# The last two row blocks of a two-stage MLP computed together, with seven products of matrix quarters in place of eight

## The reference, cut to what matters

```python
x = attention(rotate(q), rotate(k), v)      # (4, 576, 512): 4 batches, 8 heads of 64
h = x.transpose(0, 2, 1) @ U @ V            # rank 32, mixes the 576 positions
u = x + h.transpose(0, 2, 1)
ch = np.maximum(u @ w_ch1, 0.0) @ w_ch2     # 512 -> 2048 -> 512
return u + ch
```

## Time and profile before

| | us |
|---|---|
| median of 3 runs | 745.0 (744.42 to 745.64) |
| the profiled execution | 744.88 |
| its span in the profile | 743.1 |
| TensorE busy | 713.4 (96%) |
| VectorE, ScalarE, POOL busy | 405.4 (55%), 440.7 (59%), 463.5 (62%) |
| mean granted TensorE clock | 0.991 of full speed |

### The profile page before, as it was taken

How to read it: one execution, slowest core, us unless ns; L and a number is a source line. 1 busy time by engine, 2 the same in 40 slices (tenths; PEclk the granted TensorE clock), 3 DMA queues, 4 the chain that set the end, 5 groups by cost and what they waited for, 6 DMA issues and landing times.

```text
span 743.1 us, 12350 instructions
## 1 busy us (share of the span) xinstructions
PE 713.4 (96%) x4314; PEld 644.1 (87%) x4314; DVE 405.4 (55%) x677; ACT 440.7 (59%) x951; POOL 463.5 (62%) x335
## 2 busy tenths in 40 slices
PE   9899986999999999999999999899999999999997
PEld 4888875999997879999999988899899889999986
DVE  4899997555657775344444566676565441112111
ACT  2988875666767666566565665676666334333331
POOL 3999865384958664674946967639333255656563
PEclk9999997899999999999999999999999999999999
DMA  7976684528493538348274374462523253434342
GB/s 207 242 215 178 185 255 119 161 94 236 110 245 106 161 133 244 132 140 251 86 214 177 104 209 149 147 187 79 159 73 103 100 183 124 168 128 170 127 171 71
DMA packets 73757, 117.84 MB, mean 159 GB/s; under 512 B 27040, under 2 KB 27168, under 8 KB 71904
## 3 DMA queue, kind: packets, MB, share of 16 engines
q1 hardware_dynamic: 73472, 116.68, 52.2%
q10 hardware_dynamic: 224, 0.36, 0.2%
HBM read 80.15 MB, written 9.44 MB: 121 GB/s over the span
## 4 chain that ended last, share of the span: by engine, by line
PE 72%; DVE 8%; ACT 7%; POOL 6%; issue 5%; DMA 1%; POOLq 0%; SPq 0%; ACTq 0%; DVEq 0%
PE ps L1151 25%; PE ps L1167 22%; PE ps L1050 7%; PE ps L1064 7%; PE ps L1085 5%; DVE negmax L877 2%; POOL raw L588 2%; PE ps L1019 2%; ACT prob L720 2%; POOL raw L589 1%; ACT pth L731 1%; ACT w2h L784 1%; PE ps L1133 1%; ACT w1h L780 1%; POOL raw L598 1%
## 5 line engine op out<-in xcount | busy, mean ns | idle before, releaser
L655 POOL TENSOR_TENSOR w2l<-w2u,w2h 128x512 fp32r<-128x512 f32 x96 | 124.0, 1291 | 223.5 <-ACT w2h L784 223.5
L978 DVE SCALAR_TENSOR_TENSOR htl<-ps,hth 128x384 fp32r<-128x384 f32 x96 | 53.5, 558 | 177.5 <-ACT hth L791 177.0
L877 DVE TENSOR_REDUCE negmax<-ps 128x1 f32<-128x576 f32 (+1 forms) x160 | 120.2, 751 | 49.4 <-PE ps L1050 42.4
L731 ACT ACTIVATE pth<-ps 128x512 fp32r<-128x512 f32 (+1 forms) x156 | 87.7, 567 | 81.6 <-PE ps L1085 80.3
L1151 PE MATMUL ps<-ub,w1h 128*128 128x384 f32 x384 | 133.2, 347 | 1.1 <-DVE htl L978 0.6
L720 ACT ACTIVATE prob<-ps,negmax 128x576 f32<-128x576 f32 (+1 forms) x160 | 118.0, 738 | 27.3 <-DVE negmax L877 27.1
L1151 PE MATMUL ps<-ub,w1l 128*128 128x384 f32 x384 | 129.7, 338 | 0.0
L1151 PE MATMUL ps<-utl,w1h 128*128 128x384 f32 x384 | 129.5, 337 | 0.0
L649 POOL TENSOR_TENSOR w1l<-w1u,w1h 128x512 fp32r<-128x512 f32 x96 | 124.1, 1293 | 5.8 <-ACT w1h L780 5.8
L791 ACT ACTIVATE hth<-ps 128x384 fp32r<-128x384 f32 x96 | 47.0, 490 | 130.6 <-PE ps L1151 130.3
L1050 PE MATMUL ps<-stack 128*128 128x288 f32 x620 | 112.9, 304 | 7.6 <-ACT prob L720 7.2
(11 more groups left out here) (84 smaller groups left out, 1137.5 us busy)
## 6 DMA issues: line engine op xcount, KB each, us to landing
w1u<-in_w SPq DMA_DIRECT2D x96, 256.0 KB, 2.6
w2u<-in_w SPq DMA_DIRECT2D x96, 256.0 KB, 2.6
stack<-raw SPq DMA_DIRECT2D x60, 288.0 KB, 4.4
raw<-in_qk SPq DMA_DIRECT2D x14, 1152.0 KB, 5.3
stack<-raw SPq DMA_DIRECT2D x60, 144.0 KB, 4.0
v2u<-in_v SPq DMA_DIRECT2D x16, 320.0 KB, 4.2
ubu<-scratch_u SPq DMA_DIRECT2D x18, 256.0 KB, 3.6
out<-ubu SPq DMA_DIRECT2D x18, 256.0 KB, 2.4
```

What stands on the lines that cost most here:

```text
L655: nc.gpsimd.tensor_tensor(w2l[:, at], w2u[:, at], w2h[:, at], ALU.subtract).then_inc(w2_lo, 1)
L731: nc.scalar.activation(pt_of(g)[0][rows, keys, queries], source, ACT.Copy).then_inc(pt_hi, 1)
L877: nc.vector.tensor_reduce(negmax[0:WT[t], t:t + 1], scores_of(n, WT[t]), AX.XY, ALU.max, negate=True).then_inc(maxed, 1)
```

## The change

Blocks 4 and 5 are taken together, and their 16 inner blocks in HP = 8 pairs. Pair 0 is computed as before, four ups (`plain`) and the downs. In pairs 1 to 7 the 256 x 512 weights A and the 512 x 768 rows B of u are cut into 2 x 2 quarters (128 x 256 and 256 x 384), and the four up products are made from seven products of quarters and sums of quarters in place of eight, by these formulas:

- S1 = A21 + A22, S2 = S1 - A11, S3 = A11 - A21, S4 = A12 - S2 (weights, by POOL, `s_sums`, for each pair);
- T1 = B12 - B11, T2 = B22 - T1, T3 = B22 - B12, T4 = B21 - T2 (rows of u, by DVE, `sum_t`, once; they serve all seven pairs);
- P1 = A11 B11, P2 = S2 T2, P3 = A12 B21, P4 = S3 T3, P5 = S1 T1, P6 = A22 T4, P7 = S4 B22 (this is the order in which they are made);
- U2 = P1 + P2, C11 = P1 + P3, U3 = U2 + P4, C22 = U3 + P5, U4 = U2 + P5, C21 = U3 + P6, C12 = U4 + P7 (by DVE, `wide_add`).

Every product is 2 x 3 = 6 matmuls of 384 columns (`product`), and alternates between banks 5 and 7. Behind P1 to P7 stand 2, 2, 2, 2, 2, 1 and 1 downs of the pair before (`DOWNS_BEHIND`); the twelve downs of the last pair come at the end. The downs add up in six banks. ACT rounds the quarters (`round_a`, 128x768), the sums (`round_s`, 128x1024), and the T (`round_t`, 128x768 each); POOL makes the `lo` parts of quarters and sums (`a_rest`, `s_rest`), DVE those of the T (`rest_t`, 128x768 each). The relu and its `lo` part (`wide_relu`, `wide_rest`) now read C from SBUF for pairs 1 to 7; for pair 0 they read the bank. Sums, T and C lie in buffers of the attention that are free by then. Weights are loaded once for both blocks. The first pair's sums and quarters are made in slots 166 and 168. STEPS is now 64, so `MLP_REST` has three parts, the downs of step 63.

```diff
+LONE = NB - 2
+STEPS = LONE * FB
+HP = FB // 2
+PRODUCTS = ("a11", "s2", "a12", "s3", "s1", "a22", "s4")
+DOWNS_BEHIND = (2, 2, 2, 2, 2, 1, 1)
+FIRST_PAIR = NTILES + 6
...
+            def s_sums(k):
+                a21, a22, a11, a12 = (place("w_raw", k % 2, QUARTER * i, QUARTER) for i in range(4))
+                s1, s2, s3, s4 = (place("s_raw", None, QUARTER * i, QUARTER) for i in range(4))
+                pool.wait_ge(pair_loaded[k % 2], 32 * ((k + 1) // 2))
...
+                nc.gpsimd.tensor_tensor(s1, a21, a22, ALU.add).then_inc(s_sum, 1)
+                nc.gpsimd.tensor_tensor(s3, a11, a21, ALU.subtract).then_inc(s_sum, 1)
+                pool.wait_ge(s_sum, 4 * (k - 1) + 1)
+                nc.gpsimd.tensor_tensor(s2, s1, a11, ALU.subtract).then_inc(s_sum, 1)
+                pool.wait_ge(s_sum, 4 * (k - 1) + 3)
+                nc.gpsimd.tensor_tensor(s4, a12, s2, ALU.subtract).then_inc(s_sum, 1)
...
             for x in MLP_REST:
                 mlp(*x)
+            w2_rest(STEPS)
+            w2_rest(STEPS + 1)
+            for k in range(1, HP):
+                w2_rest(STEPS + 2 * k)
+                if k + 1 < HP:
+                    s_sums(k + 1)
+                    a_rest(k + 1)
+                    s_rest(k + 1)
+                w2_rest(STEPS + 2 * k + 1)
...
+            wide_relu(0, 0, 0)
+            round_w2(STEPS)
+            round_t(T3)
+            round_t(T2)
+            wide_relu(0, 0, 1)
+            wide_relu(0, 1, 0)
+            round_w2(STEPS + 1)
+            wide_relu(0, 1, 1)
+            for k in range(1, HP):
+                if k == 1:
+                    round_t(T1)
+                wide_relu(k, 0, 0)
+                if k == 1:
+                    round_t(T4)
+                round_w2(STEPS + 2 * k)
+                if k + 1 < HP:
+                    round_a(k + 1)
+                wide_relu(k, 1, 1)
+                if k + 1 < HP:
+                    round_s(k + 1)
+                wide_relu(k, 1, 0)
+                wide_relu(k, 0, 1)
+                round_w2(STEPS + 2 * k + 1)
...
+            sum_t(T3)
+            wide_rest(0, 0, 0, 1)
+            sum_t(T2)
             for x in MLP_REST:
                 mlp(*x)
+            wide_rest(0, 0, 1, 2)
+            rest_t(T3, 1)
+            rest_t(T2, 2)
+            wide_rest(0, 1, 0, 3)
+            sum_t(T1)
+            wide_rest(0, 1, 1, 4)
+            for k in range(1, HP):
+                wide_add(k, 1, "p1", None)
+                if k == 1:
+                    rest_t(T1, 3)
+                wide_add(k, 2, "u2", "p1")
+                if k == 1:
+                    sum_t(T4)
+                wide_add(k, 3, "c11", "p1")
+                if k == 1:
+                    rest_t(T4, 4)
+                wide_add(k, 4, "u3", "u2")
+                wide_rest(k, 0, 0, 1)
+                wide_add(k, 5, "c22", "u3")
+                wide_add(k, 5, "u4", "u2")
+                wide_rest(k, 1, 1, 2)
+                wide_add(k, 6, "c21", "u3")
+                wide_rest(k, 1, 0, 3)
+                wide_add(k, 7, "c12", "u4")
+                wide_rest(k, 0, 1, 4)
...
+            def product(k, j):
+                name = PRODUCTS[j]
+                if j == 0:
+                    pe.wait_ge(a_lo, k)
+                    if k == 1:
+                        pe.wait_ge(wide_lo, 3)
+                    else:
+                        pe.wait_ge(wide_sum, sums_done(k - 1, "c21"))
+                elif j == 1:
+                    pe.wait_ge(s_lo, k)
+                    if k == 1:
+                        pe.wait_ge(wide_lo, 4)
+                    else:
+                        pe.wait_ge(wide_sum, sums_done(k - 1, "c12"))
+                else:
+                    pe.wait_ge(wide_sum, sums_done(k, {2: "p1", 3: "u2", 4: "c11", 5: "u3", 6: "u4"}[j]))
...
+                for d in range(2):
+                    for q, (l, r) in enumerate(((wh, hi), (wh, lo), (wl, hi))):
+                        mm = nc.tensor.matmul(bank, l[:, P * d:P * d + P], r[:, d],
+                                              start=(d == 0 and q == 0), stop=(d == 1 and q == 2))
...
+            plain(0, 0)
             for x in MLP_REST:
                 mlp(*x)
+            plain(0, 1)
+            plain(1, 0)
+            plain(1, 1)
+            for k in range(1, HP):
+                downs = [(f, block, t) for f in range(2) for block in range(2) for t in range(TT)]
+                for j in range(HALVES):
+                    product(k, j)
+                    for _ in range(DOWNS_BEHIND[j]):
+                        wide_down(k - 1, *downs.pop(0))
+            for f in range(2):
+                for block in range(2):
+                    for t in range(TT):
+                        wide_down(HP - 1, f, block, t)
```

More of the change, by code:

```diff
@@ L233, in bank_plan, with sums_done @@
             holder[b] = tenant
-    return bank, before, left
+    return bank, before, left, {b: holder[b] for b in RING_MERGED}
+def sums_done(k, name):
+    return len(SUMS) * (k - 1) + SUMS.index(name) + 1
 def turned_in(n):
@@ L440, in res_tile, with place, two, u_part @@
         return res[:, DM * t:DM * t + DM]
+    def place(name, i=None, at=0, n=TB):
+        return place_of(name, i, at, n)
+    def two(x):
+        return x.rearrange("p (c n) -> p c n", c=2)
+    def u_part(x, d, block):
+        at = TB * ((LONE + block) % (UT // TB))
+        return x[:, 2 * d:2 * d + 2, at:at + TB]
+    def tail_bank(i, n=TB):
+        return ps[:, TAIL_UP[i] * BANK:TAIL_UP[i] * BANK + n]
+    def first_bank(k):
+        return (k - 1) % 2
+    def tail_acc(block, t):
+        return ps[:, TAIL_ACC[block][t] * BANK:TAIL_ACC[block][t] * BANK + DM]
+    def tail_res(block, t):
+        return place("res", None, DM * t, DM) if block else res_tile(t)
+    def h_part(name, k, f, block):
+        return place(name, k % 2, TB * (2 * f + block))
+    def done_before(k):
+        return 4 + HALVES * (k - 1) if k else 0
     def split_of(r):
@@ new lines, in wide_add @@
+            def wide_add(k, product, name, other):
+                dve.wait_ge(wide_done, done_before(k) + product)
+                bank = tail_bank((first_bank(k) + product - 1) % 2)
+                if other is None:
+                    if k == 1:
+                        dve.wait_ge(u_stored, 16 * NT * B)
+                        dve.wait_ge(turn_done, NT * B)
+                    nc.vector.tensor_copy(place(name), bank).then_inc(wide_sum, 1)
+                else:
+                    dve.wait_ge(wide_sum, sums_done(k, other))
+                    nc.vector.tensor_tensor(place(name), bank, place(other), ALU.add).then_inc(wide_sum, 1)
@@ L1014, in _ @@
+            for block in range(2):
+                for t in range(TT):
+                    add_rows(block, t)
         @block.tensor
@@ L1199, in _, with plain @@
                             mix(*x)
+            def plain(f, block):
+                m = 2 * f + block
+                if m == 0:
+                    pe.wait_ge(relu_lo, STEPS)
+                elif m == 1:
+                    _release(pe, last[TAIL_UP[1]], e)
+                else:
+                    pe.wait_ge(wide_lo, m - 1)
+                if block == 0:
+                    pe.wait_ge(w1_lo, STEPS + f + 1)
+                if f == 0:
+                    pe.wait_ge(ut_lo, UT_NEEDED[LONE + block])
+                at, i = TB * ((LONE + block) % (UT // TB)), STEPS + f
+                for d in range(DB):
+                    hi, lo = uth[:, d, at:at + TB], utl[:, d, at:at + TB]
+                    for q, (l, r) in enumerate(((w1h, hi), (w1h, lo), (w1l, hi))):
+                        mm = nc.tensor.matmul(tail_bank(block), l[:, i % WBUF, P * d:P * d + P], r,
+                                              start=(d == 0 and q == 0), stop=(d == DB - 1 and q == 2))
+                mm.then_inc(wide_done, 1)
@@ new lines, in wide_down @@
+            def wide_down(k, f, block, t):
+                i = STEPS + 2 * k + f
+                if t == 0:
+                    pe.wait_ge(wide_lo, 4 * k + (1 if f + block == 0 else 2 * f + block + 1 if k == 0 else 4))
+                    pe.wait_ge(w2_lo, i + 1)
+                if k == 0 and f == 0:
+                    if block == 0:
+                        pe.wait_ge(added, TT * (LONE - 1) + t + 1)
+                    elif t < 2:
+                        pe.wait_ge(expd, NTILES)
+                    else:
+                        _release(pe, last[TAIL_ACC[1][2]], e)
+                hi, lo = h_part("h_hi", k, f, block), h_part("h_lo", k, f, block)
+                for q, (l, r) in enumerate(((hi, w2h), (lo, w2h), (hi, w2l))):
+                    mm = nc.tensor.matmul(tail_acc(block, t), l[:, P * t:P * t + P], r[:, i % WBUF],
+                                          start=(k == 0 and f == 0 and q == 0), stop=(k == HP - 1 and f == 1 and q == 2))
+                if k == HP - 1:
+                    if f == 1:
+                        mm.then_inc(acc_done, 1)
```

(2 more changed lines are left out.)

206 lines of the change are left out of this document (194 added, 12 removed).

## The result

The changed kernel took 738.34 us in the median of 4 runs (737.64 to 740.78), the kernel before 745.32 (744.42 to 746.08) beside it: ratio 0.9927, 95% interval 0.9906 to 0.9948, so 5.4 us less (3.9 to 7.0); the two medians by themselves lie 7.0 us apart. Run once more in six runs against 23, it came to 740.49 against 744.47, ratio 0.9942 (0.9925 to 0.9959), 4.3 us less. The forecast was 741.8 and 3.15 us less.

What follows compares the result with a forecast made beforehand. TensorE, busy 96% of the span, was taken as the bound; 7.35 + 0.6 - 4.8 = 3.15 us gained from 744.88 gave 741.7, stated as 741.8 us. Forecast's own range 739.5 to 744.0; 8 in 10, 738.0 to 746.0.

Steps and rivals of the forecast that it cites:

- Removed matmuls: Blocks 4 and 5: 342 up matmuls on TensorE in place of 384; the 42 missing at 0.175 us gain 7.35 us.
- Rival 4: Finer alternation of products and downs costs TensorE 0.05 us a turn, 4.9 us, nothing gained: 746.7 us; chance 0.05.
- The last `w2l`: At the end, twelve downs of 8.3 us let the last `w2l` be made in time: 0.6 us gained.
- Slots 166 to 171: Preparing pair 1's sums and quarters fits into idle time of POOL and ScalarE there: no cost.
- The turn: Entry to the last two blocks: TensorE waits 4.8 us in all for VectorE, then POOL; bounds 1.3 and 7.
- The first three terms: TensorE's waits at the turn for relu `lo` parts: 1.4 us at bank 7, 1.4 at P1, 1.1 at P2.
- Pair 2: TensorE waits for POOL's `a_rest`, 0.5 us, and `s_rest`, 0.4 us, after `w2l` of step 66 waited for ScalarE.
- The steady pairs: Each pair takes 15.7 us of TensorE's work without a wait; `s_rest` has 0.4 us to spare: price 0.
- rival 2: POOL's chain is 0.9 us longer, so six pairs wait 0.5 us each, 3.0 us: 744.8 us; chance 0.2.
- Rivals 2 and 3: POOL paces the pairs; the third: 256-column sums cost 1.1 us each, 6.3 us lost, 748.0 us, chance 0.08.
- Rival 1: Meetings of POOL and VectorE don't reach TensorE; the turn costs 1.3 us: 738.2 us; chance 0.15.

Runs made afterwards that it cites:

- e4: Changed kernel with the six matmuls of the seventh product issued twice in pairs 1 to 7: 746.35 us, ratio 1.0026 to the kernel before.
- e1: The changed kernel run once more, unaltered: 740.49 us, ratio 0.9942 to the kernel before.
- e2: Changed kernel with POOL's w2 rests of steps 64 and 65 held back until certain VectorE operations are done: 738.86 us, ratio 0.9927 to before.
- e5: Changed kernel with VectorE's sums and relu rests at the turn reordered, ScalarE rounding in the same order: 737.99 us, ratio 0.9913 to before.
- e3: Changed kernel plus one unread POOL subtraction of 640 columns ahead of `s_rest` in pairs 2 to 7: 744.86 us, ratio 1.0006 to before.
- e10: Changed kernel with only ScalarE's order altered, w2 of step 66 and pair 2's quarters rounded ahead of T4: 738.4 us in one run.
- e9: The order of e5, with ScalarE also rounding w2 of step 66 and pair 2's quarters ahead of T4: 737.48 us, ratio 0.9882 to before.

## Why the prediction came out as it did

- **Removed matmuls, 7.35 us**: right. 42 fewer, and e4, which puts them back, costs 7.3 us in the stretch. The pitch does not change at the finer turns between products and downs: from the first product of pair 2 to that of pair 7 a pair takes 15.70 us in the mean ((709.16 - 630.66) / 5), 15.7 in the working. Rival 4 is out.
- **The last `w2l`, 0.6 us**: right; behind the last product the twelve downs run without a wait.
- **Slots 166 to 171, nothing**: right as far as the traces tell. The start of the stretch lies at 600.8 to 603.1 us in nine traces of the changed kernel and its variants (mean 601.5) and at 601.9 to 603.6 in three of the kernel before (mean 602.8). With a scatter of 2 us these few traces can't tell the two apart; the spans of the timed runs put both at 602.5 (see e1).
- **The turn, 4.8 us of waits**: the place, the order and the engine were right, the size too large. The first three terms, 1.4 + 1.4 + 1.1, measured 1.1 + 1.2 + 0.75. I had let successive operations of VectorE begin 0.03 us behind one another; where the next does not read what the one before wrote, it begins about 0.1 us before the other ends (the one at 613.39 began while the two from 610.55, 2.91 long together, ran to 613.46). Up to P2 these tenths sum to 0.6 us: it began 16.15 us into the stretch, in the working 16.78. The other 0.2 of the difference is TensorE's: the first matmul behind a wait costs 0.28 and 0.25 us to the next start (610.69 to 610.97, 614.08 to 614.33) in place of 0.175, which the working left out, so TensorE's own work up to P2 took 13.1 us and not 12.9.
- **Pair 2, 0.5 + 0.4 us within those 4.8**: did not happen. POOL's `a_rest` ended at 630.33, TensorE wanted it at 630.66; `s_rest` ended at 633.02, wanted at 633.11. e2 and e5 show that this was close: as soon as TensorE was 1.7 or 3.1 us earlier, the wait appeared.
- **The steady pairs, nothing, with 0.4 us to spare**: right, with more to spare, 1.1 us (e3). The relu `lo` that I had placed ahead of `s_rest` asked behind its start in pair 2 and took 2.70 us, so POOL's chain was spared one meeting; the working had named this case in rival 2. Two sizes in that working were off without changing it: POOL's next operation behind a meeting with an operation of 384 columns is late by 0.31 to 0.35 us (1.05 for 0.74 at 625.06; 0.34 in the earlier trace rows), where the chain took 0.45, which no row shows; and ScalarE's operations of a pair add up to 5.3 us, not 5.4. Rivals 2 and 3 (POOL paces the pairs) did not come; e3 is what rival 2 would have looked like.
- **Rival 1** gave 738.2, and the first median was 738.34, but not for its reason: the meetings were there and delayed TensorE by at least 1.7 us at the turn (e2 took 0.64 and 1.1 us off). That the result came so near it is luck: 738.34 lies outside the forecast's own range of 739.5 to 744.0 and only 0.3 us inside the range of 8 in 10, whose lower end was set by this rival; the 740.49 of the second session lies within both. The forecast's sum with the measured terms is 7.35 + 0.6 - 3.1 = 4.85, the 4.9 of the traces; the rest of the first difference of 7.0 us between the medians is scatter ahead of the changed part.

So the forecast was right in sign, mechanism and range, and missed 1.75 us of gain: 0.85 in the size of three waits and 0.9 in two waits that just did not occur. The 256-column POOL sums cost 0.74 us as interpolated; the first of each four is longer for a meeting (pairs 3, 5 and 7 of the kernel after, groups by line, mean ns):

```profile
L790 POOL TENSOR_TENSOR prob<-tables 128x256 f32<-128x256 f32 x3 | 3.3, 1089 | 0.0
...
L791 POOL TENSOR_TENSOR prob<-tables 128x256 f32<-128x256 f32 x3 | 2.2, 736 | 0.0
```

## What to carry to other kernels

A trick that removes matmuls is worth its full price only if the sums it needs find room on the engines that TensorE waits for; here 7.3 us were removed, and the one-time sums at the start of the new stage gave 3.1 back (1.7 of them, at least, because POOL's operations got in the way of VectorE's), of which another order of the same instructions recovered 2.4. When work is put into the queue of an engine, put it behind what releases the bottleneck and sort it by when it is wanted, and then look for the next chain: a wait removed makes the following deadline earlier, and that one had only 0.1 us to spare. Where a gain is smaller than the scatter of the rest of the kernel, compare the changed stretch from its first to its last instruction in several traces; it repeated to 0.1 us where the whole scattered by 2.

## What the runs showed of the hardware

VectorE's operations with two SBUF operands and POOL's exclude each other, and not only `tensor_tensor`: the relu `lo` parts (scalar_tensor_tensor, 0.55 us by themselves) took up to 2.70 us in the steady pairs, waiting for an `s_rest` of 2.39. In e2, where only POOL's place was changed, a sum fell from 1.59 to 0.95 us. POOL pays too: when it asks while one of VectorE's runs (1.97 for 1.29 at 604.59), and on its next operation when VectorE has asked meanwhile (1.05 for 0.74 at 625.06, behind a relu `lo`). I had not expected how much of an earlier start this takes away: POOL's chain of pair 2 began 0.7 us earlier in e10 and ended 0.1 us earlier, and began 2.2 us earlier in e9 than in e5 and ended 1.0 us earlier.
